# Weight pieces, their loads and three sums moved in a fused attention and feed-forward kernel

## The chip, the cores and the metric

The kernel runs on one core of a Trainium2 chip. The metric is the device time of one execution in microseconds. A core has TensorE (matmuls), VectorE (DVE), ScalarE (ACT), GpSimd (Pool) and SyncE (SP, which here only issues transfers), all running their own queue in order, and 16 DMA engines that they share.

## The reference

Three stages follow one another on 8 batches of 576 tokens and 512 channels. Cut to what matters:

```python
def sm_attn(qq, kk, vv):
    s = scale * np.matmul(qq, kk.transpose(0, 1, 3, 2))
    s = s - np.max(s, axis=-1, keepdims=True)
    a = np.exp(s)
    a = a / (np.sum(a, axis=-1, keepdims=True) + 1e-09)
    return np.matmul(a, vv)
p_packed = sm_attn(p, k, v)              # 32 packed rows per head
x = sm_attn(q, p_packed, p_packed)       # (8, 576, 512) after heads are joined
...
xk = mu_k * x + (1.0 - mu_k) * x_prev    # x_prev: x moved by one token
xr = mu_r * x + (1.0 - mu_r) * x_prev
k = np.maximum(xk @ w_k, 0.0)            # 512 -> 1024
x = 1.0 / (1.0 + np.exp(-(xr @ w_r))) * (k * k @ w_v)
...
h = xt @ U @ V                           # over tokens, rank 32
u = x + h.transpose(0, 2, 1)
out = u + np.maximum(u @ w_ch1, 0.0) @ w_ch2   # 512 -> 2048 -> 512
```

## The kernel before

Every matrix product is done in three passes on a high and a low part of each operand (`_hi`, `_lo`): ScalarE writes the high part, VectorE (for the first weights, Pool) subtracts it to get the low part.

**First part, four groups of three chunks (`chunk_plan`).** A chunk is 384 tokens and has 17 places, its slots: eight k groups (L778), three r groups (L757) and six halves of three v groups (L792), each of twelve matmuls. The batches' attention is laid between them at numbered places. Around them go the mix and split of the next chunk, and for each of the three token tiles of a chunk its split (`x2s`, L868 on ScalarE and L872 on VectorE) and its sum over tokens with U (`g`, L861 on TensorE); `g_evac` takes the sum out. The last group of three chunks (kind LAST) has no attention. It has the transposes of u (`u`), their parts (`us`) and, from `PIECE_ITEMS`, the first 20 weight pieces.

**Weight pieces.** The second layer's weights are needed as seven combinations for a Strassen-like product (`NPROD` = 7, 32 pieces of 128 x 1024 numbers). A piece is loaded into `piece_raw` or `late_raw` (L1210 to L1216, by Pool), Pool makes four sums (L1222 to L1227, `pool_piece`), ScalarE writes the high parts (`ws_hi`, L1248), VectorE the low parts (`ws_lo`, L1253), and SyncE stores 896 KB (`ws_store`, L1345) into `w_parts`. The 20 early pieces have three slots and lie in LAST; `b_loads` waits until they are all stored and then loads V, the sums g and the x tiles. The 12 late ones have two slots and lie in the first half pass of the second part.

**Second part (`pair_plan`).** Five pairs of column blocks, each in two halves g with two layers: 28 products of the first (`m1`, L1036, in order e = 7i + pos) and 28 of the second (`m2`, L1118, e from 28). A product is six matmuls. SyncE loads 256 KB of `w_parts` for each of them into an eleven-deep ring (L1365), which waits for the product 11 before. For the second layer ScalarE (L1136) and VectorE (L1142) split the hidden values three products ahead.

**What sets the order.** It is written out: `first_items`, `chunk_plan`, `pair_plan` give one list of items, and each engine takes from it, in this order, what is its own. So an item's place in the list is its place in the queue of every engine that it uses. Pool alone has its own loop. A late piece is converted at the spots of `LATE_SPOTS`; at each spot come first the store of the piece two before, then the split of the one before, then the conversion:

```python
    for kind, after in (("ws_store", 2), ("ws_lo", 1), ("ws_hi", 0)):
```

**Start.** SyncE issues p, then k's first two parts, then q of batch 0; ScalarE issues k's other two and v. `WEIGHTS_AFTER` puts conversions of the first part's ten weight chunks (`w`) behind attention steps; chunks 0 to 3 are w_k, 4 and 5 w_r, 6 to 9 w_v. Line numbers below are those of the profile of this kernel.

## Time and profile before

| | us |
|---|---|
| median of three runs | 1506.16 (1502.21 to 1509.39) |
| profiled execution | 1503.87 |
| its span | 1501.2 |
| TensorE matmul busy | 1342.2 (89%) |
| VectorE busy | 946.9 (63%) |
| ScalarE busy | 699.6 (47%) |
| Pool busy | 228.6 (15%) |

The granted TensorE clock was 0.959 of full speed on the mean. The span runs from the first to the last instruction; 2.7 us lie around it. Busy shares are a mean over stages with different limits, so the stretches of the rows below are read one by one: attention and the first layer to 693.7 us (the last group of chunks from 531.4), the second part from there on.

### The profile page before, as it was taken

How to read it: one execution, taken by the hardware profiler on the slowest of the kernel's cores; microseconds unless marked ns; L12 is line 12 of the kernel's file. 1: busy time of each engine (PE TensorE's matmuls, PEld its weight loads, DVE VectorE, ACT ScalarE, POOL GpSimd, SP SyncE). 2: the span in 40 equal slices, each digit the busy share in tenths (PEclk: the TensorE clock that was granted, in tenths of full speed). 3: DMA queues.
4: the chain of work that ended last, by engine and by line, in shares of the span. 5: the costliest groups of instructions: out<-in, count | busy, mean ns of one | idle time of the engine just before them, and what ended most of it. 6: DMA issues, size and time to landing. Idle time of an engine off the chain costs nothing.

```text
span 1501.2 us, 21219 instructions
## 1 busy us (share of the span) xinstructions
PE 1342.2 (89%) x7592; PEld 1139.1 (76%) x7592; DVE 946.9 (63%) x1549; ACT 699.6 (47%) x1240; POOL 228.6 (15%) x294
## 2 busy tenths in 40 slices
PE   2379999999999997799666999999999999899997
PEld 1268787788878886587444878888788879799996
DVE  2666668666676756636444486756866586467756
ACT  1445465454445553544322454445544554355543
POOL 2700000000000049813432020001100010011000
PEclk9589999999999999899877999999999999999999
DMA  7733243333322048764855757876687668977986
GB/s 149 175 79 73 67 87 80 80 56 75 73 66 59 8 136 272 233 212 139 273 172 184 241 166 212 235 210 205 174 245 217 204 186 245 256 243 237 265 275 163
DMA packets 372454, 252.47 MB, mean 168 GB/s; under 512 B 249280, under 2 KB 286176, under 8 KB 372352
## 3 DMA queue, kind: packets, MB, share of 16 engines
q1 hardware_dynamic: 361056, 235.58, 55.9%
q0 software_dynamic: 4960, 13.79, 3.0%
q10 hardware_dynamic: 6336, 1.77, 0.5%
q8 instruction: 61, 1.00, 0.3%
q14 instruction: 41, 0.34, 0.1%
HBM read 201.25 MB, written 49.81 MB: 167 GB/s over the span
## 4 chain that ended last, share of the span: by engine, by line
PE 68%; DVE 11%; DMA 6%; SPq 4%; POOL 4%; issue 3%; ACT 3%; ACTq 0%; DVEq 0%; POOLq 0%
PE bank L1036 22%; PE bank L1118 19%; PE bank L778 11%; PE bank L792 7%; PE bank L757 3%; SPq L1288 3%; DVE mixed L730 2%; DMA w_parts<-late_out 2%; DVE hid_parts L1142 2%; DMA w_ring<-w_parts 2%; PE bank L861 1%; PE bank L931 1%; ACT mixed L717 1%; DMA late_raw<-in_moe_w_ch 1%; DVE acc L1161 1%
## 5 line engine op out<-in xcount | busy, mean ns | idle before, releaser
L1118 PE MATMUL bank<-hid_parts,w_ring 128*128 128x512 f32 (+1 forms) x1680 | 373.9, 381 | 41.8 <-DVE hid_parts L1142 30.1
L1118 PEld LDWEIGHTS bank<-hid_parts,w_ring 128*128 128x128 f32 x1680 | 312.2, 194 | 101.9 <-issue 53.8
L1036 PE MATMUL bank<-u_parts,w_ring 128*128 128x512 f32 (+1 forms) x1680 | 357.6, 370 | 13.8 <-ACT hid_raw L1046 6.8
L1036 PEld LDWEIGHTS bank<-u_parts,w_ring 128*128 128x128 f32 x1680 | 307.2, 189 | 54.4 <-issue 15.3
L1142 DVE TENSOR_TENSOR hid_parts<-hid_raw,hid_parts 128x512 fp32r<-128x512 f32 (+1 forms) x280 | 186.5, 673 | 97.0 <-ACT hid_parts L1136 93.6
L1136 ACT ACTIVATE hid_parts<-hid_raw 128x512 fp32r<-128x512 f32 (+1 forms) x280 | 163.2, 587 | 145.4 <-PE bank L1118 142.5
L778 PE MATMUL bank<-xk_hi,wk_hi 128*128 128x384 f32 x384 | 133.4, 347 | 13.5 <-DVE xk_lo L749 8.9
L778 PE MATMUL bank<-xk_lo,wk_hi 128*128 128x384 f32 x384 | 130.9, 341 | 0.0
L778 PE MATMUL bank<-xk_hi,wk_lo 128*128 128x384 f32 x384 | 130.8, 341 | 0.0
L792 PE MATMUL bank<-wv_hi,k_hi 128*128 128x512 f32 x288 | 116.2, 404 | 0.4 <-DVE k_lo L828 0.4
L792 PE MATMUL bank<-wv_lo,k_hi 128*128 128x512 f32 x288 | 114.9, 399 | 0.0
L792 PE MATMUL bank<-wv_hi,k_lo 128*128 128x512 f32 x288 | 114.3, 397 | 0.0
L835 DVE TENSOR_TENSOR square<-square 128x384 f32<-128x384 f32 x96 | 55.3, 576 | 88.6 <-ACT square L812 88.2
L812 ACT ACTIVATE square<-bank 128x384 f32<-128x384 f32 x96 | 46.9, 488 | 114.3 <-PE bank L778 100.9
L1070 DVE TENSOR_TENSOR hid_raw<-bank,hid_raw 128x512 f32<-128x512 f32 (+1 forms) x40 | 25.5, 638 | 112.0 <-PE bank L1036 112.0
L778 PEld LDWEIGHTS bank<-xk_hi,wk_hi 128*128 128x128 f32 x384 | 73.8, 192 | 23.0 <-issue 13.9
L1161 DVE TENSOR_TENSOR acc<-bank,acc 128x512 f32<-128x512 f32 (+1 forms) x140 | 86.4, 629 | 7.2 <-PE bank L1118 6.9
L730 DVE SCALAR_TENSOR_TENSOR mixed<-x,mu,mixed 128x384 f32<-128x384 f32 x96 | 58.2, 668 | 42.5 <-ACT mixed L717 42.4
L960 POOL TENSOR_TENSOR u_sums<-acc 128x512 f32<-128x512 f32 (+1 forms) x10 | 11.7, 1179 | 449.2 <-ACT acc L949 449.2
L1059 ACT ACTIVATE hid_raw<-hid_raw 128x512 f32<-128x512 f32 (+1 forms) x80 | 46.9, 587 | 61.7 <-DVE hid_raw L1070 44.4
L778 PEld LDWEIGHTS bank<-xk_lo,wk_hi 128*128 128x128 f32 x384 | 73.9, 192 | 1.0
L778 PEld LDWEIGHTS bank<-xk_hi,wk_lo 128*128 128x128 f32 x384 | 73.8, 192 | 0.0
(155 smaller groups left out, 1921.7 us busy)
## 6 DMA issues: line engine op xcount, KB each, us to landing
w_ring<-w_parts SPq DMA_DIRECT2D x560, 256.0 KB, 3.7
w_parts<-piece_out SPq DMA_DIRECT2D x20, 896.0 KB, 5.0
w_parts<-late_out SPq DMA_DIRECT2D x12, 896.0 KB, 5.5
x_scratch<-x SPq DMA_DIRECT2D x36, 256.0 KB, 2.0
kq_parts<-in_k SPq DMA_DIRECT2D x120, 72.0 KB, 2.6
kq_parts<-in_q SPq DMA_DIRECT2D x112, 72.0 KB, 2.2
v_rows<-in_v SPq DMA_DIRECT2D x56, 128.0 KB
out_dram<-acc SPq DMA_DIRECT2D x84, 64.0 KB, 3.0
```

The costliest lines, as they stand in the source:

```text
L730: last = nc.vector.scalar_tensor_tensor(out3, segments(c, ft, 0), mu[:, which, ft:ft + 1], out3, ALU.mult, ALU.add)
L757: last = nc.tensor.matmul(bank, a, b_, start=(done == 0), stop=(done == 3 * n_terms - 1))
L778: last = nc.tensor.matmul(bank[:, 0:CHUNK], wk[a][:, ct, at * P:(at + 1) * P], xk[b_][:, ct, :], start=(ct == 0 and a == 0 and b_ == 0), s ...
L792: last = nc.tensor.matmul(bank, k2[a][:, f, at * P:(at + 1) * P], wv[b_][:, f, :], start=(f == 0 and a == 0 and b_ == 0), stop=(f == NFA - ...
L812: nc.scalar.activation(square[:, at % 2, :], bank[:, 0:CHUNK], ACT.Relu).then_inc(k_ev, 1)
L835: nc.vector.tensor_tensor(square[:, at % 2, :], square[:, at % 2, :], square[:, at % 2, :], ALU.mult).then_inc(squared, 1)
L1036: last = nc.tensor.matmul(to, wring[:, e % RW, ct, a, :], uc[:, pos, b, ct, 0:w], start=(pos in FRESH and ct == 0 and a == 0 and b == 0), ...
L1059: nc.scalar.activation(h, h, ACT.Relu).then_inc(relu_ok, 1)
L1118: last = nc.tensor.matmul(role(st, j, BANK_OF[pos])[:, 0:w], wring[:, e % RW, j, a, :], hid[:, no % RH, b, 0:w], start=(pos in FRESH and i ...
L1136: nc.scalar.activation(hid[:, no % RH, 0, 0:w], raw[:, pos, i, 0:w], ACT.Copy).then_inc(hid_hi, 1)
L1142: nc.vector.tensor_tensor(hid[:, no % RH, 1, 0:w], raw[:, pos, i, 0:w], hid[:, no % RH, 0, 0:w].bitcast(F32), ALU.subtract).then_inc(hid_l ...
L1161: nc.vector.tensor_tensor(to, role(st, j, name)[:, 0:w], to, ALU.add).then_inc(sum_ok, 1)
```

## The change

- The 12 late pieces are placed four products apart from e = 3 on: conversion at e, split and store at e + 1. Before, they stood at 14 spots three to five products apart, conversion, split and store one spot after the other.
- The 20 early pieces stand at 3 + 9n/5 instead of 4 + 7n/5, their stores two places after the conversion instead of three, and SyncE issues their loads (`ws_load`) instead of Pool, two pieces ahead. The late pieces are still loaded by Pool, one ahead.
- The sum g of tile 3c+1 moves from the end of its chunk to behind the second k group of the next; the split of tile 3c-1 and its sum go one to three places later. In the last chunk `b_loads`, `b_v`, `u` and `us` start one place later.
- At the start Pool issues the first p load (with a semaphore of its own), ScalarE issues v after the second and the fourth part of k have landed, weight chunks 4 and 5 are converted after the first mix, and Pool's low part of chunk 4 waits for the split of the first mix.

```diff
@@ -74,7 +74,7 @@
...
-WEIGHTS_AFTER = {"scores2": 1, "sm1": 3, "norm1": 2}
+WEIGHTS_AFTER = {"scores2": 1, "sm1": 3}
@@ -126,9 +126,13 @@
...
         items.append(slot)
-        if at == (2 if c == 2 else 0) and (c > 0 or kind != FIRST):
+        if at == (4 if c == 2 else 2) and (c > 0 or kind != FIRST):
             items.append(("x2s", 3 * c - 1, 0) if c > 0 else ("x2s", 8, -1))
-        if c == 2 and at == 1:
+        if at == 1 and (c > 0 or kind != FIRST):
+            items.append(("g", 3 * c - 2, int(c == 0), 0) if c > 0 else ("g", 7, 1, -1))
+            if c == 2:
+                items.append(("g_evac", 0, 0))
+        if c == 2 and at == 3:
             items.append(("g", 4, 1, 0))
@@ -136,16 +140,12 @@
...
                 items += loads_after(n, step)
-        if at == 4 and c == 0 and kind != FIRST:
+        if at == 5 and c == 0 and kind != FIRST:
             items += [("g", 8, 1, -1), ("g_evac", 1, -1)]
-        if at == 3 + c and c > 0:
+        if at == (5 if c == 1 else 7) and c > 0:
             items.append(("g", 3 * c - 1, c - 1, 0))
...
             items.append(("g", 3 * c, int(c == 2), 0))
-        if at == NSLOT - 1:
-            items.append(("g", 3 * c + 1, int(c == 2), 0))
-            if c == 1:
-                items.append(("g_evac", 0, 0))
         if not last_chunk:
@@ -160,11 +160,10 @@
...
-            items += {4: [("b_loads",)], 6: [("b_v",)], 7: [("u", 0, 0), ("u", 0, 1)], 8: [("u", 0, 2), ("u", 0, 3)],
-                      9: [("u", 0, 4), ("u", 0, 5), ("b_ring",)], 10: [("u", 0, 6), ("u", 0, 7)],
-                      11: [("us", 0, 0), ("us", 0, 1)], 12: [("us", 0, 2), ("us", 0, 3)], 13: [("us", 0, 4), ("us", 0, 5)],
-                      14: [("us", 0, 6), ("us", 0, 7)], 15: [("us", 0, 8), ("us", 0, 9), ("us", 0, 10)],
-                      16: [("us", 0, 11), ("us", 0, 12), ("us", 0, 13)]}.get(at, [])
+            us = lambda *ks: [("us", 0, k) for k in ks]
+            items += {5: [("b_loads",)], 7: [("b_v",)], 8: [("u", 0, 0), ("u", 0, 1)], 9: [("u", 0, 2), ("u", 0, 3)],
+                      10: [("u", 0, 4), ("u", 0, 5), ("b_ring",)], 11: [("u", 0, 6), ("u", 0, 7)],
+                      12: us(0, 1), 13: us(2, 3), 14: us(4, 5, 6), 15: us(7, 8, 9), 16: us(10, 11, 12, 13)}.get(at, [])
     return items
@@ -195,10 +194,14 @@
...
     for n in range(PIECES - LATE):
-        at = 4 + 7 * n // 5
+        at = 3 + 9 * n // 5
+        if n == 0:
+            plan.setdefault(0, []).extend([("ws_load", m) for m in range(SLOTS_P)])
+        elif n + SLOTS_P - 1 < PIECES - LATE:
+            plan.setdefault(at, []).append(("ws_load", n + SLOTS_P - 1))
         plan.setdefault(at, []).append(("ws_hi", n))
         plan.setdefault(at + 1, []).append(("ws_lo", n))
-        plan.setdefault(at + 3, []).append(("ws_store", n))
+        plan.setdefault(at + 2, []).append(("ws_store", n))
     return plan
@@ -230,22 +233,18 @@
...
-LATE_SPOTS = [(0, 1, 1), (0, 1, 5), (0, 2, 2), (0, 2, 6), (0, 3, 1), (0, 3, 5)] + [(1, 0, e) for e in range(3, 19, 3)] + [(1, 0, 21), (1, 0, 24)]
+def late_items(e):
+
+
+    n, rest = divmod(e - 3, 4)
+    if e < 3 or n >= LATE or rest > 1:
+        return []
+    n += PIECES - LATE
+    return [("ws_hi", n)] if rest == 0 else [("ws_lo", n), ("ws_store", n)]
...
 TURN_AT = (5, 11, 17, 23)
-
-
-def late_pieces(spot):
-
-
-    at = LATE_SPOTS.index(spot)
-    items = []
-    for kind, after in (("ws_store", 2), ("ws_lo", 1), ("ws_hi", 0)):
-        if 0 <= at - after < LATE:
-            items.append((kind, PIECES - LATE + at - after))
-    return items
@@ -256,8 +255,9 @@
...
                 items.append(("m1", g, i, pos))
-                if p == 0 and g == 0 and i == 0 and pos < 3:
-                    items += [[("x2s", 8, PAIRS - 1)], [("g", 8, 1, PAIRS - 1)], [("g_evac", 1, PAIRS - 1)]][pos]
+                if p == 0 and g == 0 and i == 0 and pos < 4:
+                    items += [[("g", 7, 1, PAIRS - 1)], [("x2s", 8, PAIRS - 1)], [("g", 8, 1, PAIRS - 1)],
+                              [("g_evac", 1, PAIRS - 1)]][pos]
                 if i > 0 and pos < 2:
@@ -267,8 +267,8 @@
...
                     items += turns.pop(0)
-                if p == 0 and g == 0 and (0, i, pos) in LATE_SPOTS:
-                    items += late_pieces((0, i, pos))
+                if p == 0 and g == 0:
+                    items += late_items(NPROD * i + pos)
                 if g == 0 and i == 1 and pos == 0 and p < NB - 1:
@@ -282,8 +282,8 @@
...
             items.append(("m2", g, pos, i))
-            if p == 0 and g == 0 and (1, 0, e) in LATE_SPOTS:
-                items += late_pieces((1, 0, e))
+            if p == 0 and g == 0:
+                items += late_items(NPROD * NU + e)
             if g == 0 and e in TURN_AT and turns:
@@ -356,7 +356,7 @@
...
         self.z_early_in = [sem(f"z_early_in{i}") for i in range(KQ - ZS)]
-        self.p_in, self.v_in = sem("p_in"), sem("v_in")
+        self.p_first_in, self.p_in, self.v_in = sem("p_first_in"), sem("p_in"), sem("v_in")
         self.kq_ok, self.p_scaled, self.pT_ok = sem("kq_ok"), sem("p_scaled"), sem("pT_ok")
@@ -1199,7 +1199,7 @@
...
-    def load_piece(pool, n):
+    def load_piece(eng, n):
@@ -1207,13 +1207,13 @@
...
             rows = w1.rearrange("(k c p) f -> p c k f", k=2, c=2, p=P)[:, half, :, :]
-            pool.dma_start(r[:, 1:5:3, :], rows[:, :, fa:fa + P]).then_inc(piece_in[slot], 16)
-            pool.dma_start(r[:, 0:8:7, :], rows[:, :, fb:fb + P]).then_inc(piece_in[slot], 16)
+            eng.dma_start(r[:, 1:5:3, :], rows[:, :, fa:fa + P]).then_inc(piece_in[slot], 16)
+            eng.dma_start(r[:, 0:8:7, :], rows[:, :, fb:fb + P]).then_inc(piece_in[slot], 16)
         else:
             cols = lambda f: w2[f:f + P, :].rearrange("p (k j n) -> p j k n", k=2, j=2)[:, half, :, :]
-            pool.dma_start(r[:, 1, :], cols(fa)[:, 0, :]).then_inc(piece_in[slot], 16)
-            pool.dma_start(r[:, 0, :], cols(fa)[:, 1, :]).then_inc(piece_in[slot], 16)
-            pool.dma_start(r[:, 4:8:3, :], cols(fb)).then_inc(piece_in[slot], 16)
+            eng.dma_start(r[:, 1, :], cols(fa)[:, 0, :]).then_inc(piece_in[slot], 16)
+            eng.dma_start(r[:, 0, :], cols(fa)[:, 1, :]).then_inc(piece_in[slot], 16)
+            eng.dma_start(r[:, 4:8:3, :], cols(fb)).then_inc(piece_in[slot], 16)
@@ -1226,15 +1226,15 @@
...
-    def pool_pieces(pool, first, end, slots):
-        for n in range(first, first + slots - 1):
-            load_piece(pool, n)
-        for n in range(first, end):
+    def late_pieces(pool):
+        first = PIECES - LATE
+        load_piece(pool, first)
+        for n in range(first, PIECES):
             pool_piece(pool, n)
-            if n + slots - 1 < end:
+            if n + 1 < PIECES:
                 if n > first:
                     pool.wait_ge(piece_lo, n)
-                load_piece(pool, n + slots - 1)
+                load_piece(pool, n + 1)
@@ -1292,7 +1292,7 @@
...
             src = p[n, hp:H:2, :, 32 * dh:32 * dh + 32].rearrange("c n d -> n c d")
-            eng.dma_start(att.pz[32 * quad:32 * quad + 32, :, :], src).then_inc(att.p_in, 16)
+            eng.dma_start(att.pz[32 * quad:32 * quad + 32, :, :], src).then_inc(att.p_in if n else att.p_first_in, 16)
@@ -1328,7 +1328,6 @@
...
-                load_p(sp, 0)
                 for i in range(CT // 2):
@@ -1414,6 +1413,13 @@
...
                     load_ring(e)
+            elif item[0] == "ws_load":
+                if item[1] < SLOTS_P:
+                    sp.wait_ge(att.x_act, 2 * B)
+                    sp.wait_ge(att.x_dve, 2 * B)
+                else:
+                    sp.wait_ge(piece_lo, item[1] - SLOTS_P + 1)
+                load_piece(sp, item[1])
             elif item[0] == "ws_store":
@@ -1461,9 +1467,13 @@
...
-            pool.wait_ge(att.p_in, 64 * (n + 1))
+            if n:
+                pool.wait_ge(att.p_in, 64 * n)
+            else:
+                pool.wait_ge(att.p_first_in, 64)
             nc.gpsimd.tensor_scalar(att.pz[:, :, :], att.pz[:, :, :], SCALE, None, ALU.mult).then_inc(att.p_scaled, 1)
...
+        load_p(pool, 0)
         for i, m in enumerate((mu_k, mu_r)):
@@ -1485,6 +1495,8 @@
...
             pool.wait_ge(w_hi, i + 1)
+            if i == CT:
+                pool.wait_ge(x_lo, 2)
             nc.gpsimd.tensor_tensor(dst[1], parts(stage_a[i % RA], a), dst[0].bitcast(F32),
@@ -1497,13 +1509,14 @@
...
         pool.wait_ge(att.x_dve, 2 * B)
-        pool_pieces(pool, 0, PIECES - LATE, SLOTS_P)
+        for n in range(PIECES - LATE):
+            pool_piece(pool, n)
         pieces_stored(pool)
...
         pool.wait_ge(u_lo, 2 * NPROD)
-        pool_pieces(pool, PIECES - LATE, PIECES, 2)
+        late_pieces(pool)
         for p in range(1, NB):
@@ -1553,6 +1566,8 @@
...
                     load_z(act, 0, i)
+                act.wait_ge(att.z_in[CT // 2 - 1], 64)
+                act.wait_ge(att.z_in[CT - 1], 64)
                 load_v(act, 0)
```

The order on ScalarE in the second layer of the first half pass; late_out is the conversion of a late piece, hid_parts a split. Before:

```order
L1248 ACTIVATE late_out<-late_raw 128x7x128
L1136 ACTIVATE hid_parts<-hid_raw 128x512 x3
L1248 ACTIVATE late_out<-late_raw 128x7x128
L1136 ACTIVATE hid_parts<-hid_raw 128x512 x3
L1248 ACTIVATE late_out<-late_raw 128x7x128
L1136 ACTIVATE hid_parts<-hid_raw 128x512 x3
L1248 ACTIVATE late_out<-late_raw 128x7x128
L1136 ACTIVATE hid_parts<-hid_raw 128x512 x7
```

And now:

```order
L1248 ACTIVATE late_out<-late_raw 128x7x128
L1136 ACTIVATE hid_parts<-hid_raw 128x512 x4
L1248 ACTIVATE late_out<-late_raw 128x7x128
L1136 ACTIVATE hid_parts<-hid_raw 128x512 x4
L1248 ACTIVATE late_out<-late_raw 128x7x128
L1136 ACTIVATE hid_parts<-hid_raw 128x512 x6
```

Four splits instead of three stand between two conversions, and six instead of seven behind the last.

The order on SyncE in the middle of the early pieces, where pieces of w2 are stored: piece_raw is a load, w_parts<-piece_out a store, x_scratch the store of a token tile. Before, where the loads were Pool's:

```order
L1345 DMA w_parts<-piece_out 896x1x256 [waits piece_lo] x2
L1397 DMA x_scratch<-x 128x512 [waits x2_ok]
L1345 DMA w_parts<-piece_out 896x1x256 [waits piece_lo]
L1345 DMA w_parts<-piece_out 128x7x256 [waits piece_lo] x8
L1397 DMA x_scratch<-x 128x512 [waits x2_ok]
```

And now:

```order
L1396 DMA x_scratch<-x 128x512 [waits x2_ok]
L1344 DMA w_parts<-piece_out 896x1x256 [waits piece_lo]
L1214 DMA piece_raw<-in_moe_w_ch 128x128 [waits piece_lo]
L1215 DMA piece_raw<-in_moe_w_ch 128x128
L1216 DMA piece_raw<-in_moe_w_ch 128x2x128
L1344 DMA w_parts<-piece_out 128x7x256 [waits piece_lo]
L1214 DMA piece_raw<-in_moe_w_ch 128x128 [waits piece_lo]
L1215 DMA piece_raw<-in_moe_w_ch 128x128
L1216 DMA piece_raw<-in_moe_w_ch 128x2x128
```

A load stands behind the store of an earlier piece in one queue.

The order on ScalarE at the start, from the second exp of batch 0 on; wk_hi, wr_hi and wv_hi are the weight conversions, x the copy of the attention's result. Before:

```order
L1563 ACTIVATE wk_hi<-stage_x 128x1024
L1563 ACTIVATE wr_hi<-stage_x 128x1024
L1563 ACTIVATE wr_hi<-stage_r 128x1024
L607 ACTIVATE x<-bank 128x2x288 x2
L717 ACTIVATE mixed<-x,one_minus_mu 128x384 x4
L742 ACTIVATE xk_hi<-mixed 128x768 x2
L1563 ACTIVATE wv_hi<-stage_r 128x1024 x2
```

And now:

```order
L1578 ACTIVATE wk_hi<-stage_x 128x1024
L607 ACTIVATE x<-bank 128x2x288 x2
L717 ACTIVATE mixed<-x,one_minus_mu 128x384 x4
L742 ACTIVATE xk_hi<-mixed 128x768 x2
L1578 ACTIVATE wr_hi<-stage_x 128x1024
L1578 ACTIVATE wr_hi<-stage_r 128x1024
L1578 ACTIVATE wv_hi<-stage_r 128x1024 x2
```

The two conversions of w_r moved behind the copies, the mix and its split.

## Rows read from the trace of the kernel before

**Rows 1.** Stretches: length, busy us by engine, PEclk, DMA share, GB/s.

```profile
577.00:642.20 65.20, 51.68 (x230) 43.40 (x230) 43.33 (x51) 30.33 (x50) 53.06 (x76) 0.92 0.78 252
531.40:693.70 162.30, 140.78 (x675) 121.32 (x674) 92.99 (x125) 77.61 (x136) 89.55 (x130) 0.95 0.60 196
693.70:829.40 135.70, 95.44 (x338) 74.17 (x339) 62.88 (x85) 43.23 (x70) 49.32 (x80) 0.84 0.69 216
```

**Rows 2.** Chain that ended last: start us, length, engine, output and line.

```profile
81.75 2.09 DVE mixed L730 x4
...
386.36 10.43 PE bank L778 x60
...
959.03 33.09 PE bank L1118 x144
```

**Rows 3.** Waits, of 693-830, 545-642, 531-694, 185-545: total, times, longest.

```profile
ACT late_out L1248 <- DMA w_parts<-late_out: 63.5, 9, 8.7
...
ACT piece_out L1248 <- POOL piece_raw L1227: 42.1, 15, 4.9
...
PE bank L861 <- DVE x2s_lo L872: 13.8, 3, 6.4
...
PE bank L861 <- DVE x2s_lo L872: 6.6, 3, 3.2
```

**Rows 4.** Timeline of Pool, late pieces: start, length, what, [idle before <- releaser].

```profile
695.64 0.72 POOL L1210 DMA_DIRECT2D late_raw<-in_moe_w_ch  x1 [6.26 <-DVE u_parts L999]
...
702.00 0.72 POOL L1210 DMA_DIRECT2D late_raw<-in_moe_w_ch  x1
...
735.33 0.45 POOL L1222 TENSOR_TENSOR late_raw<-late_raw 128x128 f32<-128x128 f32 x1 [2.98 <-DMA late_raw<-in_moe_w_ch]
...
790.43 0.56 POOL L1214 DMA_DIRECT2D late_raw<-in_moe_w_ch  x1
...
797.39 0.60 POOL L1222 TENSOR_TENSOR late_raw<-late_raw 128x128 f32<-128x128 f32 x1 [5.17 <-DMA late_raw<-in_moe_w_ch]
...
800.52 0.55 POOL L1214 DMA_DIRECT2D late_raw<-in_moe_w_ch  x1
```

**Rows 5.** Early pieces: Pool's timeline, then landing times of stores and loads.

```profile
596.55 0.55 POOL L1214 DMA_DIRECT2D piece_raw<-in_moe_w_ch  x1
...
601.43 0.55 POOL L1214 DMA_DIRECT2D piece_raw<-in_moe_w_ch  x1
...
DMA to landing us min/median/max: 4.2/5.3/8.6
...
DMA to landing us min/median/max: 2.6/4.0/5.3
```

**Rows 6.** Last chunk: timeline of SyncE and TensorE, then landing of x_tiles.

```profile
643.97 0.52 SPq L1345 DMA_DIRECT2D w_parts<-piece_out  x1
...
651.59 0.52 SPq L1382 DMA_DIRECT2D x_tiles<-x_scratch  x1
...
660.14 0.66 PE L931 MATMUL bank<-ident,x_tiles 128*128 128x128 f32 x4 [0.34 <-DVE v L1658]
...
DMA to landing us min/median/max: 5.3/6.5/7.7
```

**Rows 7.** Timeline of the start, all engines.

```profile
6.25 10.15 ACTq L1302 DMA_DIRECT2D v_rows<-in_v  x8
...
17.73 0.71 DVE L632 STREAM_TRANSPOSE kqT<-kq_parts 128x512 f32<-128x512 f32 x1 [6.53 <-DMA kq_parts<-in_k]
...
23.52 0.74 ACT L588 ACTIVATE probs<-bank,neg_max 128x576 f32<-128x576 f32 x1 [2.98 <-DVE neg_max L650]
...
49.67 17.79 SPq L1288 DMA_DIRECT2D kq_parts<-in_k  x16
...
54.70 5.67 DVE L730 SCALAR_TENSOR_TENSOR mixed<-x,mu,mixed 128x384 f32<-128x384 f32 x4 [1.38 <-ACT mixed L717]
...
70.55 1.77 PE L533 MATMUL bank<-kqT,pT 64*32 64x288 f32 x32 [3.43 <-DVE pT L646]
```

## The prediction

> **What bounds the kernel now.** I read the busy time by stretch first. The last group of three chunks (531.4 to 693.7 us) and the first half of the first pass of the second layer (693.7 to 829.4 us) are where TensorE is not full: 140.8 of 162.3 us and 95.4 of 135.7 us, at a granted clock of 0.95 and 0.84 [rows 1]. The chain of waits gives the undisturbed pace: five k groups in 10.43 us, and 144 matmuls of 512 columns in 33.09 us, 0.230 us each [rows 2]. So a chunk of eight k groups and nine groups of twelve 512-column matmuls needs 8 x 2.09 + 9 x 2.76 = 41.5 us and some 1.4 us for three sums, 43 us; three chunks and some 6 us for the transposes of u make 135 us, and the stretch loses 27 us, of which the middle chunk alone (577 to 642, 65.2 us) loses 22. The half pass needs 56 products x 6 x 0.230 = 77 us and loses 58 us.
>
> The waits say why. ScalarE runs in order, and its conversion of a weight piece (L1248) waits: 63.5 us in 9 waits, up to 8.7 us each, for the store of the piece two before it, and 42.1 us in 15 waits for Pool's sums of the piece [rows 3]. Behind it stand ScalarE's evacuations and splits, without which TensorE has no operand or no bank. The x2s waits of TensorE in these chunks (13.8 us, 3 times) come from the same stall; between 185 and 545 us they are 6.6 us.
>
> **Late pieces (12, in the half pass).** Before, piece n's store is issued two places after its conversion, and the conversion of n+2, which needs the same slot, stands right behind it. So every piece pays a landing, 7 us of ScalarE's time on the mean. After, the store stands one product after the conversion and the slot is wanted eight products later; this wait goes. What is late next is Pool: it loads one piece ahead, and issue, landing and four sums follow one another on it. From 695.64 to 702.00 us that took 6.4 us for the first piece; for a w2 piece it took 10.1 us (790.43 to 800.52), made of 1.8 of issue, 5.17 of waiting for the landing and 3.1 of sums [rows 4]. In the lightest case of the same rows the landing leaves 2.98 us of waiting, and a sum takes 0.45 us. Lower bound of the period: 1.8 + 3.0 + 1.8 = 6.6 us; upper bound 10.1. After the change the store of a piece starts some 2 us behind the next load instead of ahead of it, and VectorE is idle when ScalarE waits, so I take 1.8 + 4.2 + 2.4 = 8.4 us. Four products at full speed take 5.5 us, so Pool, not TensorE, sets the pace.
> End of the half pass: first sums done at 702.0; three more w1 pieces at 6.7, 722; eight w2 pieces x 8.4, 789; a conversion, its latency and nine products, 14, gives 803 instead of 829.4: **-26 us** (bounds: period 10.1 gives 817, -12; 6.6 gives 789, -41). A check by bytes: the stage moves 135.7 us x 216 GB/s = 29.3 MB [rows 1]; in 109 us this is 268 GB/s, more than the 252 GB/s which the busiest chunk held for 65 us, so there is little room below 8 us.
>
> **Early pieces (20, in the last three chunks).** Their loads leave Pool for SyncE. Pool's cycle was 4.88 us (596.55 to 601.43) [rows 5], with 1.8 of issue in it; it becomes some 3.1 us, while the pieces come every 1.8 places instead of 1.4: 3.7 us among k groups, 4.9 among r and v. The Pool wait should nearly go, and the x2s waits behind it. I leave 7 us of stall of the 27. Now SyncE has each load behind the store of an earlier piece and behind the waits of the x stores. Nobody else is queued there but the stores themselves; a load has two pieces, over 7 us, of lead.
> The Trainium skill (DMA: Bandwidth & Descriptors, Issuing engines are not separate DMA queues) says that DMAs from all engines share 16 DMA engines, and that another issuing engine saves only issue time. By that rule the move is worth the 1.8 us on Pool and nothing in transfer; a landing is not made shorter by it. The trace cannot show it before the change.
> The price comes at the end. The last piece is stored at place 39 instead of 33, and the loads for the second layer wait until all pieces are stored. Before: store at 643.97, x_tiles issued at 651.59, 7.6 us later, landing 6.5 us, and TensorE's first use at 660.14, some 2 us after that [rows 6]. After: four more k groups and the conversion put the last store 14 us behind the chunk's start (642.2 in the trace); +7.6 + 6.5 gives 28 us behind it, while its use stands 20.7 us behind it (660.14 - 642.2 and one r group more). TensorE waits 7 to 8 us, and restarts slowly; I take 9. With 1 us for the tighter splits of u: 27 - 7 - 9 - 1 = **-10 us**. The other way round: the first piece is split 8 us after 531.4, the last one 20 periods later, then come 14 us to x_tiles and 31 us to the first product (660.14 to 693.7, one r group less). With today's 4.88 us that is 8 + 98 + 45 = 151 us, 11 less than now. Bounds: -20 (2 us of stall in the chunks, 6 at the end, no more) and +3 (5.6 us a piece, 165 us).
>
> **Middle sums.** The sums of tile 3c+1 move from the end of a chunk behind the second k group of the next, and the splits two places later. Nothing is added; ScalarE's and VectorE's work is the same. Of the 6.6 us of [rows 3] and a little before 185 us I take **-5**, bounds 0 and -7: VectorE's attention steps can be as late at the new place.
>
> **Start.** The v loads of batch 0 now wait on ScalarE until two z loads have landed, and its first exp is queued behind them. Eight of the ten took 10.15 us to issue, so some 13 us in all [rows 7]. The last k of batch 0 was there at 17.73 with v's packets beside it; without them I take 13. Then ScalarE is free near 26 instead of 19, and exp starts at some 27 instead of 23.52: +3.5. The first p load moves to Pool, whose next work waits anyway. Against it: one weight conversion that waited for its DMA stood before the copy of x (-1.6), and the mix took 5.67 us for four operations while Pool worked beside it, against 2.09 at 81.75 [rows 2] (-3.5). What Pool now does later still ends before its reader.
> The Trainium skill (SBUF — State Buffer, Who interferes with whom) says that a VectorE operation with two SBUF inputs and a GpSimd operation that reads SBUF lock each other out. The row agrees, and by the rule the whole 3.5 us are won at that place.
> But TensorE then meets batch 1's scores, which wait for its k; they start at 70.55, three us behind the end of k's issue on SyncE (49.67 + 17.79) [rows 7]. That issue stands behind batch 0's q and batch 1's v, and v waits for batch 0's pv, which comes 2 to 4 us later. So the gain is not seen at all, and the loss partly, as the transfers still have the same bytes to move: **+1 us**, bounds -4 and +5.
>
> **Sum.** -26 - 10 - 5 + 1 = -40. The profiled execution took 1503.87 us (span 1501.2, 2.7 around it); it becomes 1464. The median before, 1506.16, is 2.3 above it, so I predict 1465 to 1466: **1465 us**.
>
> **The rivals.** A, Pool's late cycle stays at 10.1 us because loads and stores still meet: -12 instead of -26, **1479**. For it: the last five w2 pieces all had it. Against: in those the store was issued first.
> B, the late pieces run at 6.6 us: -41 instead of -26, **1450**. For it: the light landings. Against: the bytes, 29.3 MB in 95 us, 308 GB/s.
> C, slower than before. SyncE's queue serialises the early pieces: store landing 5.3, then the load behind it 4.0 [rows 5], sums 3.1 to 4, conversion and split 2.3, is 15.2 us a round. With three pieces a round that is 5.1 us, near today's. If only two are in flight (load n+2 is issued beside conversion n) it is 7.6 us a piece: 8 + 152 + 45 = 205 us for the stretch instead of 162. That is +43 - 26 - 5 + 1 = +13, **1519**. It decides from some 7 us a piece. Against it: three slots, and the load needs only the split of piece n-1.
> D, no change to be told: all bounds on the bad side at once, -12 + 3 + 0 + 5 = -4, **1502**.
> By the Trainium skill (DMA: Bandwidth & Descriptors, Queues, rings and completion order) a ring is consumed in order, and different rows take turns; that speaks for C's mechanism, since the load now shares the store's row.
>
> **How the numbers follow.** Forecast 0.52 (its own range 1453 to 1478: late period 7.6 to 9.3 us is -32 to -19, early stretch 5 either way); A 0.20; B 0.16; C 0.06; D 0.06. The range 1443 to 1490 leaves out C, D and a rest of B. A measurement of this kernel tells 0.5% (7.5 us) from no change. Faster by more: forecast, A and B, 0.88. Within: D, 0.06. Slower: C, 0.06.
>
> **What would show it.** Right: ScalarE's wait for late_out on the stores gone, in its place a wait for Pool's late sums of some 3 us a piece; late conversions 8 to 9 us apart; the second half of the pass starting some 26 us sooner behind the first product; the middle chunk of the last group near 47 us; TensorE waiting once, 5 to 10 us, for x_tiles; the first scores of batch 1 within 3 us of 70.55. Wrong: conversions at 6 or at 10 us (B, A); ScalarE still waiting for Pool in the early pieces, with Pool waiting for a load behind a store (C); a start more than 5 us away.

## The result and the profile after

| | before | after |
|---|---|---|
| median of the executions | 1506.20 us | 1462.90 us |
| lowest and highest | 1502.21 to 1509.39 | 1459.35 to 1465.13 |
| span of the profiled execution | 1501.2 us | 1463.1 us |

The ratio after to before is 0.9712, with a 95% interval from 0.9681 to 0.9742: 2.9% faster, 43.3 us by the medians. The forecast was 1465 us. The two profiled executions stand 38.1 us apart: that of before lies under its median, that of after over its own (it took 1465.13 us).

The sum came out well, but two of its four terms did not. I go through the stretches first. The columns are length, busy us of PE, PEld, VectorE, ScalarE and GpSimd, granted clock, DMA share and GB/s. In the kernel after, the last three chunks one by one (each from its first k product to that of the next, the third up to the first product of the second layer), then the half pass up to the first product of the second half:

```profile
537.87:580.50 42.63, 42.63 (x211) 37.82 (x210) 31.34 (x41) 24.53 (x42) 23.77 (x32) 1.00 0.64 198
580.50:624.89 44.39, 42.89 (x211) 37.74 (x210) 35.30 (x46) 26.21 (x44) 26.29 (x39) 1.00 0.86 272
624.89:688.79 63.90, 52.04 (x258) 45.23 (x256) 26.31 (x40) 26.57 (x49) 18.58 (x21) 0.91 0.56 184
688.79:792.90 104.11, 87.15 (x340) 66.04 (x341) 61.02 (x86) 44.01 (x70) 44.87 (x80) 0.94 0.90 290
```

The kernel before, cut at the same instructions:

```profile
530.87:582.81 51.94, 44.54 (x211) 38.67 (x210) 31.06 (x44) 25.34 (x44) 31.16 (x52) 0.93 0.56 183
582.81:642.01 59.20, 47.34 (x211) 40.20 (x210) 38.35 (x47) 27.87 (x46) 47.35 (x70) 0.91 0.76 245
642.01:693.70 51.69, 49.43 (x258) 42.98 (x256) 24.01 (x37) 24.39 (x47) 11.55 (x10) 1.00 0.47 150
```

With [rows 1] for the half pass of before, the account is: the first two chunks 24.1 us shorter (51.94 + 59.20 against 42.63 + 44.39), the third 12.2 us longer, the half pass 31.6 us shorter; and all of it starts 7.0 us later than before (537.87 against 530.87). Part of the gain shows as a higher granted clock: TensorE's busy time fell by 6.4 us in the first two chunks (0.93 and 0.91 before, 1.00 now) and by 8.3 us in the half pass (0.84 before, 0.94 now), for about the same number of matmuls. These rows also correct the cut of the prediction: it let the middle chunk begin at 577, but its first k product is at 582.8. The loss of 27 us over the three chunks stands; it lay 9 us in the first and 16 us in the middle one, not 22 in the middle.

What ScalarE waits for in the half pass (689 to 793) and in the last three chunks (537 to 689), and TensorE between 185 and 530 us; columns: total, times, longest. They answer to [rows 3].

```profile
ACT late_out L1248 <- POOL late_raw L1227: 29.8, 11, 5.4
...
ACT piece_out L1248 <- POOL piece_raw L1227: 22.6, 11, 3.3
...
PE bank L861 <- DVE x2s_lo L872: 6.6, 3, 3.2
```

The 63.5 us in which a late conversion waited for a store are gone; in their place stand 29.8 us for GpSimd's late sums. GpSimd's timeline shows that round, as [rows 4] did before (start, length, what; in the fences below also, in brackets, the idle time ahead of it and its releaser):

```profile
697.30 0.72 POOL L1210 DMA_DIRECT2D late_raw<-in_moe_w_ch  x1
...
721.49 0.57 POOL L1214 DMA_DIRECT2D late_raw<-in_moe_w_ch  x1
...
774.33 0.56 POOL L1214 DMA_DIRECT2D late_raw<-in_moe_w_ch  x1
```

From 721.49 to 774.33 lie seven w2 pieces: 52.84 / 7 = 7.55 us each. From 697.30 to 721.49 lie three w1 pieces: 8.06 us each.

The last chunk answers to [rows 6]; SyncE and TensorE there:

```profile
640.51 0.51 SPq L1344 DMA_DIRECT2D w_parts<-piece_out  x1
...
646.75 1.16 SPq L1385 DMA_DIRECT2D g<-g_scratch  x2
648.02 0.52 SPq L1381 DMA_DIRECT2D x_tiles<-x_scratch  x1
...
654.52 1.09 PE L931 MATMUL bank<-ident,x_tiles 128*128 128x128 f32 x4 [8.65 <-DMA g<-g_scratch]
```

And the start, all engines, as [rows 7]:

```profile
10.34 9.84 ACTq L1302 DMA_DIRECT2D v_rows<-in_v  x8
...
13.07 2.18 PE L533 MATMUL bank<-kqT,pT 64*32 64x288 f32 x32 [13.07 <-DVE pT L646]
...
24.38 0.74 ACT L588 ACTIVATE probs<-bank,neg_max 128x576 f32<-128x576 f32 x1
...
30.49 2.36 PE L550 MATMUL bank<-v_rows,probs 128*32 128x64 f32 x80 [2.83 <-DMA v_rows<-in_v]
...
55.03 4.43 DVE L730 SCALAR_TENSOR_TENSOR mixed<-x,mu,mixed 128x384 f32<-128x384 f32 x4 [1.38 <-ACT mixed L717]
...
72.36 4.67 POOL L1500 TENSOR_TENSOR wv_lo<-stage_x,wv_hi 128x1024 fp32r<-128x1024 f32 x2
...
72.98 4.94 DVE L835 TENSOR_TENSOR square<-square 128x384 f32<-128x384 f32 x2
73.11 2.17 PE L533 MATMUL bank<-kqT,pT 64*32 64x288 f32 x32 [5.43 <-DVE pT L646]
...
79.30 0.74 ACT L588 ACTIVATE probs<-bank,neg_max 128x576 f32<-128x576 f32 x1 [1.29 <-DVE neg_max L650]
```

The z loads of batch 0 (here the parts of k) now land first, and the first scores start at 13.07 us instead of 20.46. But the first exp starts at 24.38, later than before, pv (the product with v) at 30.49 instead of 26.73, and batch 1's scores at 73.11. The last sum of x in the first chunk starts at 137.34 us instead of 131.42. GpSimd's last weight part, VectorE's squares and batch 1's exp in the kernel before, for comparison with the last rows:

```profile
66.97 4.64 POOL L1488 TENSOR_TENSOR wv_lo<-stage_x,wv_hi 128x1024 fp32r<-128x1024 f32 x2
...
70.42 2.08 DVE L835 TENSOR_TENSOR square<-square 128x384 f32<-128x384 f32 x2
...
73.88 0.74 ACT L588 ACTIVATE probs<-bank,neg_max 128x576 f32<-128x576 f32 x1 [1.29 <-DVE neg_max L650]
```

### The profile page after: what moved, and what is told of

The parts are those of the page before. It is cut to its first block, busy times and chain, and to the rows that moved or that the text cites. A ratio compares the mean times of both kernels' runs of the same rounds, so it can differ in the third digit from the quotient of the medians.

```text
span 1463.1 us, 21223 instructions
## 1 busy us (share of the span) xinstructions
PE 1332.2 (91%) x7592; PEld 1130.9 (77%) x7592; DVE 944.6 (65%) x1549; ACT 700.4 (48%) x1240; POOL 200.3 (14%) x250
## 4 chain that ended last, share of the span: by engine, by line
PE 64%; DVE 13%; DMA 9%; SPq 4%; POOL 3%; issue 3%; ACT 2%; ACTq 1%; DVEq 0%; POOLq 0%
PE bank L1036 21%; PE bank L1118 18%; PE bank L778 9%; PE bank L792 7%; PE bank L757 4%; DMA late_raw<-in_moe_w_ch 4%; DVE mixed L730 2%; DMA w_ring<-w_parts 2%; SPq L1288 1%; DVE hid_parts L1142 1%; PE bank L931 1%; DVE square L835 1%; DVE u_parts L999 1%; SPq L1302 1%; DMA piece_raw<-in_moe_w_ch 1%
## 5 line engine op out<-in xcount | busy, mean ns | idle before, releaser
L1118 PE MATMUL bank<-hid_parts,w_ring 128*128 128x512 f32 (+1 forms) x1680 | 361.4, 371 | 20.2 <-DVE hid_parts L1142 11.4
L1118 PEld LDWEIGHTS bank<-hid_parts,w_ring 128*128 128x128 f32 x1680 | 301.6, 188 | 78.5 <-issue 33.9
L835 DVE TENSOR_TENSOR square<-square 128x384 f32<-128x384 f32 x96 | 59.0, 616 | 80.3 <-ACT square L812 80.1
```

The lines of the kernel that those rows point to most:

```text
L835: nc.vector.tensor_tensor(square[:, at % 2, :], square[:, at % 2, :], square[:, at % 2, :], ALU.mult).then_inc(squared, 1)
L1118: last = nc.tensor.matmul(role(st, j, BANK_OF[pos])[:, 0:w], wring[:, e % RW, j, a, :], hid[:, no % RH, b, 0:w], start=(pos in FRESH and i ...
```

## The experiments

My theory after the two traces: each of the four parts of the change works in its own stretch, and they add up, -32, -12, 0 and +5 or 6 us. The rival: the parts are entangled (a faster clock, other transfers, a sum moved by another edit). So first each part was undone alone. The times of before in these runs had medians of 1504.7 to 1506.6 us, so that medians can be compared across runs.

### Late pieces undone

```diff
-                if p == 0 and g == 0:
-                    items += late_items(NPROD * i + pos)
+                if p == 0 and g == 0 and (0, i, pos) in LATE_SPOTS:
+                    items += late_pieces((0, i, pos))
```

> The changed kernel with the twelve late pieces back at their old places (store two places behind the conversion, the next conversion of the slot right behind it); all else as changed. Read from the two traces, the late half pass lost 31.5 of its 136.6 us, so the local theory gives 1462.9 + 31.5 = 1494, with ScalarE's waits for the stores back at some 60 us. The prediction's own term (26) gives 1489. The rival is that part of the 31.5 us is the gift of something else (the faster clock of a fuller stretch before, or loads of the second layer that now come in another order): then under 20 us come back, 1482 or less.

Measured: 1495.81 us, ratio to before 0.9933 (0.991 to 0.9957). That is 32.9 us more than the changed kernel. Its half pass, and ScalarE's wait in it:

```profile
684.05:821.18 137.13, 96.84 (x340) 75.07 (x341) 63.04 (x86) 43.36 (x70) 49.68 (x80) 0.84 0.68 215
```

```profile
ACT late_out L1252 <- DMA w_parts<-late_out: 62.7, 9, 8.7
```

The stretch is back at its old length, clock and wait, with the chunks ahead of it still in their new form. The late term is 33 us and comes from this edit alone.

### Early pieces undone

```diff
-        at = 3 + 9 * n // 5
+        at = 4 + 7 * n // 5
...
-        for n in range(PIECES - LATE):
-            pool_piece(pool, n)
+        pool_pieces(pool, 0, PIECES - LATE, SLOTS_P)
```

with the stores, the loads on GpSimd and the places of u as before.

> The changed kernel with the twenty early pieces back as before: their loads on GpSimd, 1.4 places apart, store three places behind, and u of the last chunk one place sooner. Read from the traces, the last three chunks went from 162.3 to 149.9 us: 12.4 us should come back, 1475. The prediction's term (10) gives 1473. The rival: the last three chunks gained because the sums of the middle tile moved, not by the pieces; then less than 5 us come back here and the 12 us appear in the run with the sums undone.

Measured: 1478.25 us, ratio 0.9819 (0.9789 to 0.9849), 15.4 us more than the changed kernel. In its own trace the last three chunks take 164.7 us (539.43 to 704.10) against 150.9, that is 13.8 us; the cut above, against the kernel before, gave 11.9 (24.1 less 12.2). The differences are within the intervals. ScalarE's wait for GpSimd's sums is 42.7 us in 15 waits again.

### Early loads back on GpSimd, places as changed

```diff
-        elif n + SLOTS_P - 1 < PIECES - LATE:
-            plan.setdefault(at, []).append(("ws_load", n + SLOTS_P - 1))
...
+        pool_pieces(pool, 0, PIECES - LATE, SLOTS_P)
```

> The changed kernel with one part of the early pieces' edit undone: their loads are issued by GpSimd again, two pieces ahead; the places of conversions, splits and stores stay as changed (1.8 places apart). Undoing the whole edit cost 15.3 us (1478.3 against 1462.9). Theory 1, what was won is GpSimd's time (1.8 us of issue in a round of 4.9): most of it goes again, 1472 to 1478, and ScalarE waits for the sums as long as before (some 40 us). Theory 2, it is the wider spacing, and the queue that issues is of no account: 1463 to 1466. In between tells the shares.

Measured: 1470.38 us, ratio 0.9761 (0.974 to 0.9782): 7.5 us of the 15.4 go again. ScalarE's wait in the last three chunks, here and below it in the kernel with the whole part undone:

```profile
ACT piece_out L1244 <- POOL piece_raw L1223: 32.7, 15, 3.9
```

```profile
ACT piece_out L1245 <- POOL piece_raw L1224: 42.7, 15, 5.0
```

42.7 us with both undone, 32.7 with the new places, 22.6 with the new places and SyncE: each half of the edit takes 10 us off the wait and some 7.5 off the time. In the traces the three chunks take 164.7, 159.0 and 150.9 us. Neither theory alone was right; the shares are about equal. (The half called places holds the earlier stores and the later u too.) That the move to another queue bought GpSimd's issue time, 1.8 us a piece, fits this but is argued, and it is not the whole of it, for GpSimd now waits more for landings: 2.6 us in 4 waits with the loads in its own queue, and in the changed kernel (the window takes in the wait for the first piece of all)

```profile
POOL piece_raw L1222 <- DMA piece_raw<-in_moe_w_ch: 165.6, 14, 130.0
```

so that 35.6 us in 13 waits remain beside the first, of 130.0.

### Middle sums undone

```diff
-        if at == (4 if c == 2 else 2) and (c > 0 or kind != FIRST):
+        if at == (2 if c == 2 else 0) and (c > 0 or kind != FIRST):
...
+        if at == NSLOT - 1:
+            items.append(("g", 3 * c + 1, int(c == 2), 0))
```

> The changed kernel with the middle tile's sums and the splits of x2 at their old places. By the prediction's term (5 us won) it would take 1468. By the trace, where the milestones between 185 and 530 us drifted by +1.5 us and the waits for x2s there stayed at 6.6 us in 3 waits, the move is worth nothing in that stretch: 1461 to 1463, unless the last three chunks need it.

Measured: 1462.12 us, ratio 0.971 (0.9682 to 0.9737), 0.8 us less than the changed kernel: nothing. The last sum of x in two successive chunks, first the changed kernel, then this one:

```profile
245.98 0.69 DVE L846 TENSOR_TENSOR x<-bank,x 128x512 f32<-128x512 f32 x1 [0.77 <-PE bank L792]
...
297.56 0.69 DVE L846 TENSOR_TENSOR x<-bank,x 128x512 f32<-128x512 f32 x1 [0.54 <-PE bank L792]
```

```profile
245.36 0.69 DVE L845 TENSOR_TENSOR x<-bank,x 128x512 f32<-128x512 f32 x1 [2.16 <-PE bank L791]
...
296.05 0.69 DVE L845 TENSOR_TENSOR x<-bank,x 128x512 f32<-128x512 f32 x1 [0.54 <-PE bank L791]
```

And its wait for x2s from 185 to 530 us:

```profile
PE bank L860 <- DVE x2s_lo L871: 6.6, 3, 3.2
```

The chunk takes 51.58 us with the move and 50.69 without (before: 50.68); the same 0.9 us shows again at the next middle group. From the last sum of x in the first chunk to that in the ninth, 400.7 us pass with the move and 400.9 without it, so even this is made up elsewhere. The waits of TensorE for x2s from 185 to 530 us are 6.6 us in 3 waits in all three kernels: the move did not touch the waits it was credited with.

### Start undone, and its wait alone

```diff
-WEIGHTS_AFTER = {"scores2": 1, "sm1": 3}
+WEIGHTS_AFTER = {"scores2": 1, "sm1": 3, "norm1": 2}
...
-            if i == CT:
-                pool.wait_ge(x_lo, 2)
...
-                act.wait_ge(att.z_in[CT // 2 - 1], 64)
-                act.wait_ge(att.z_in[CT - 1], 64)
```

with the first p load on SyncE again. In the second kernel only the last two lines are taken out.

> The changed kernel with the start as before: weight parts in their old order, no wait of ScalarE for z ahead of the v loads, no wait of GpSimd for x_lo, first p load on SyncE. By the prediction's term (+1) it takes 1462. By the traces the third tile of the first chunk was summed at 137.3 instead of 131.4 us and the lag stayed: undoing it gives 6 us, 1457. The rival: the lag is made up later by slack elsewhere, and nothing is won.

> The changed kernel without ScalarE's two waits for z ahead of the v loads of batch 0; the other edits of the start stay. Undoing all of the start took 5.2 us off (1457.7 against 1462.9). Theory 1, the wait is the cost: nearly all comes back, 1458, the first exp starts when the scores are there (within 3 us of their end), pv near 27 us. Theory 2, the cost is in the order of the weight parts and GpSimd's wait for x_lo, which is still running when batch 1's k is wanted: 1462 to 1463.

Measured: 1457.72 us, ratio 0.9681 (0.9652 to 0.9711), with the whole start undone; 1458.71 us, ratio 0.9693 (0.9672 to 0.9715), with the wait alone taken out. The start costs 5.2 us and 4.2 of them are the wait, by medians whose intervals reach 3 to 5 us to either side. The rows show where the time goes. The second kernel:

```profile
68.32 4.64 POOL L1500 TENSOR_TENSOR wv_lo<-stage_x,wv_hi 128x1024 fp32r<-128x1024 f32 x2
...
71.86 1.99 DVE L835 TENSOR_TENSOR square<-square 128x384 f32<-128x384 f32 x2
71.99 2.18 PE L533 MATMUL bank<-kqT,pT 64*32 64x288 f32 x32 [9.00 <-DVE pT L646]
...
75.23 0.74 ACT L588 ACTIVATE probs<-bank,neg_max 128x576 f32<-128x576 f32 x1 [1.29 <-DVE neg_max L650]
```

Batch 1's scores come only 1.1 us sooner than in the changed kernel, but the exp behind them 4.1 us sooner (75.23 against 79.30). Between them stands VectorE's pair of squares: 1.99 us here, 4.94 in the changed kernel, where GpSimd's wv_lo runs from 72.36 to 77.03 beside it. In this kernel wv_lo ends at 72.96. The pair ends 0.9 us behind the end of wv_lo in both (77.92 and 73.85). So of the 4.1 us at that exp, 1 is the direct cost of the wait, by the later v, k and scores, and 3 come because GpSimd's weight parts are moved into the way of VectorE. That these 4.1 us are the 4.2 of the time is not shown: single traces scatter by more between there and the end of the chunk (see what is still open).

### v of batch 0 on GpSimd, in two places

```diff
-                act.wait_ge(att.z_in[CT // 2 - 1], 64)
-                act.wait_ge(att.z_in[CT - 1], 64)
-                load_v(act, 0)
...
+        pool.wait_ge(att.z_in[CT // 2 - 1], 64)
+        pool.wait_ge(att.z_in[CT - 1], 64)
+        load_v(pool, 0)
```

> The changed kernel with the v loads of batch 0 issued by GpSimd, behind the first p load and the same two waits for z, instead of by ScalarE. ScalarE is then free when the scores of batch 0 are there. If the loss of the start is ScalarE's queue behind the wait, and not the order of the packets, the first exp starts near 17 to 18 us instead of 24.4, pv follows v's landing near 22 to 25 instead of 30.5, and the loss of 5.2 us goes with a gain of some 2 more: 1455 to 1458. If it is the packets of v, which land as late as before, pv stays near 30 and the time at 1462.

> As the run with v's loads on GpSimd, but placed behind the scaling of the first p, which there stood behind them and held back the first scores to 22.2 us. If ScalarE's queue is what the wait costs, the scores start near 13, the first exp near 16 to 17, pv as soon as v has landed, 24 to 27 instead of 30.5, and the time is 1454 to 1458. If the start is bound by the bytes (batch 1's k and the weights are behind v in any case), the scores and exp come sooner and the time stays at 1461 to 1463.

Measured: 1461.57 us, ratio 0.9707 (0.9688 to 0.9727), where v's loads stand ahead of GpSimd's small loads and its scaling of p; the scores started at 22.23 us only, since the scaling of p was queued behind v. My expectation of an exp at 17 us fell by that, and the run did not test what it was meant to. With the loads behind the scaling: 1457.98 us, ratio 0.9677 (0.9654 to 0.9699). Its start:

```profile
16.03 0.74 ACT L592 ACTIVATE probs<-bank,neg_max 128x576 f32<-128x576 f32 x1 [8.53 <-DVE neg_max L654]
...
66.51 4.66 POOL L1507 TENSOR_TENSOR wv_lo<-stage_x,wv_hi 128x1024 fp32r<-128x1024 f32 x2
...
67.81 4.24 DVE L839 TENSOR_TENSOR square<-square 128x384 f32<-128x384 f32 x2
...
73.44 0.74 ACT L592 ACTIVATE probs<-bank,neg_max 128x576 f32<-128x576 f32 x1 [1.29 <-DVE neg_max L654]
```

With nothing else queued behind the wait, the order z before v brings everything forward at first: scores at 12.96, exp at 16.03, pv at 24.95, and the issue of batch 1's k starts at 45.81 instead of 51.60. But the squares are still caught behind wv_lo (4.24 us), and the time equals that of the old start: no gain over it is shown.

### Late loads on SyncE, two pieces ahead

```diff
-    return [("ws_hi", n)] if rest == 0 else [("ws_lo", n), ("ws_store", n)]
+    return [("ws_hi", n)] if rest == 0 else [("ws_lo", n), ("ws_load", n + 2), ("ws_store", n)]
...
-            if n + 1 < PIECES:
-                if n > first:
-                    pool.wait_ge(piece_lo, n)
-                load_piece(pool, n + 1)
```

> The changed kernel with the loads of the twelve late pieces issued by SyncE, two pieces ahead (each behind the split of the piece two before it), so that GpSimd only sums. Theory 1, GpSimd's serial round (issue, landing, sums: 7.55 us by the trace) sets the late pace: the period falls to TensorE's four products, 5.5 to 6 us, and the half pass from 105 to some 90 us, 1448 to 1450. Theory 2, the bytes set it (29.3 MB in 105 us is 279 GB/s already): the period stays over 7 us, 1457 to 1463, and GpSimd waits as long for landings as before.

Measured: 1447.97 us, ratio 0.9622 (0.9604 to 0.964), 14.9 us less than the changed kernel. The half pass, ScalarE's waits for a late conversion, and the page's line on the late stores (KB each, median us to landing):

```profile
686.52:778.35 91.83, 83.39 (x341) 66.00 (x342) 62.02 (x86) 45.09 (x70) 29.61 (x48) 0.95 0.98 328
```

```profile
ACT late_out L1244 <- DMA w_parts<-late_out: 5.5, 2, 5.0
ACT late_out L1244 <- POOL late_raw L1229: 4.1, 3, 2.2
```

```profile
w_parts<-late_out SPq DMA_DIRECT2D x12, 896.0 KB, 7.2
```

The stretch is 12.3 us shorter, and ScalarE's wait for GpSimd falls from 29.8 to 4.1 us. GpSimd's first sums of the eight w2 pieces lie between 721.0 and 764.6 us, 6.2 us apart. Theory 1 holds, if with a period of 6.2 us where it said 5.5 to 6: the serial round on GpSimd set the late pace, not the bytes. The rate rose to 328 GB/s over the stretch; a late store now lands after 7.2 us instead of 5.2, a late load after 4.2 instead of 3.8. Here the Trainium skill (DMA: Bandwidth & Descriptors, Issuing engines are not separate DMA queues) fits what was seen: another engine saves issue time and no transfer time. The landings got longer, not shorter, and the gain is the round that GpSimd no longer has to serve one step after the other. The run changes two things at once, the queue that issues and the lead (two pieces instead of one); no run parts them.

### 22 early pieces instead of 20

```diff
-LATE = 12
+LATE = 10
...
-        at = 3 + 9 * n // 5
+        at = 3 + 8 * n // 5
```

> The changed kernel with 22 pieces in the last three chunks and 10 in the half pass, instead of 20 and 12: the early ones stand 1.6 places apart instead of 1.8, and end at the same place. By the trace two late pieces of 7.55 us go, 15 us; an early round of GpSimd is near 3.1 us and two more should cost 0 to 6 us: 1448 to 1454. The rival: the early stretch is at its limit too (in which case ScalarE waits for GpSimd's sums there again, by more than the present 22.6 us), and gives back 10 us or more: 1458 or above.

Measured: 1469.68 us, ratio 0.9774 (0.9746 to 0.9801), 6.8 us more. The time is the rival's (1458 or above), and so is ScalarE's longer wait. The three chunks and the half pass, then two waits in the chunks:

```profile
534.53:694.31 159.78, 138.98 (x677) 121.09 (x676) 91.56 (x127) 79.12 (x137) 65.62 (x98) 0.95 0.68 217
694.31:792.87 98.56, 86.33 (x340) 66.81 (x341) 59.05 (x84) 42.12 (x68) 38.55 (x68) 0.93 0.89 282
```

```profile
ACT piece_out L1248 <- POOL piece_raw L1227: 31.2, 12, 5.7
...
PE bank L861 <- DVE x2s_lo L872: 8.6, 2, 6.9
```

The chunks take 159.8 us instead of 150.9, the half pass 98.6 instead of 104.1. That is 3.3 us of the 6.8; the profiled execution is this kernel's fastest (1465.34 us) and enters the chunks 3.3 us sooner than that of the changed kernel. My expectation of 15 us less there was reckoned wrongly: without a late piece its four products still take 5.5 us, so that a piece costs 7.55 - 5.5 = 2 us, and two of them 4. With pieces 1.6 places apart GpSimd waits 47.7 us in 13 waits for landings (35.6 in 13 in the changed kernel), ScalarE waits longer for the sums, and TensorE again waits up to 6.9 us for x2s. The spacing of 1.8 is near the edge.

### The two best together, and three products apart

> The changed kernel with the late pieces' loads on SyncE, two ahead (15 us won alone), and the start as before (5 us won alone). The two stretches are over 500 us apart, so the two should add up: 1448.0 - 5.2 = 1443. If the lag of the start is partly absorbed later on, 1446 to 1448.

Measured: 1443.30 us, ratio 0.9584 (0.9559 to 0.9608): the two gains add up to within a us. This kernel beats both. In it the late pieces were then set three products apart:

```diff
-    n, rest = divmod(e - 3, 4)
+    n, rest = divmod(e - 3, 3)
```

> The kernel of the run before (late loads on SyncE, start as before, 1443.3 us) with the twelve late pieces three products apart instead of four. There the period ran at 5.5 to 7 us with 350 to 380 GB/s moved, where the changed kernel moved 280 to 335. Theory 1, the transfers are now what binds: the pieces come no faster, TensorE only waits sooner, 1441 to 1446. Theory 2, four products of 5.5 us still set the pace: the pieces end some 10 us sooner and the half pass, which is still 10 us over its unhindered 77, gives back 3 to 8: 1435 to 1440.

Measured: 1456.20 us, ratio 0.967 (0.9647 to 0.9693), 12.9 us slower; both theories missed the size and the second the sign. The half pass has 10.5 us of it. That stretch, the same of the kernel it was made from, and the wait that came back:

```profile
678.03:777.87 99.84, 85.83 (x340) 67.05 (x341) 63.62 (x86) 44.57 (x70) 29.33 (x48) 0.91 0.93 302
```

```profile
681.12:770.42 89.30, 81.47 (x341) 63.98 (x341) 61.37 (x86) 44.81 (x70) 29.65 (x48) 0.98 0.99 337
```

```profile
ACT late_out L1244 <- DMA w_parts<-late_out: 16.7, 6, 5.8
```

Two slots three products apart leave six products for conversion, split and landing of a store, eight before. ScalarE stands in its queue for the store again, 16.7 us, as it did in the kernel before with 63.5.

## Why the prediction was right, and where it was not

**Late pieces: -26 predicted, -31.6 in the trace, -32.9 by undoing.** The mechanism was the one forecast: the wait for the store vanished, and a wait for GpSimd's sums took its place, 29.8 us over 11 pieces, 2.7 each (some 3 forecast). Mis-sized was the period: 8.4 us predicted, 7.55 measured for w2, eight of them 7 us less. Two smaller errors largely cancel each other: the three w1 pieces took 8.06 instead of 6.7 us (+4), the tail from the last sums to the second half 11.3 instead of 14 (-3). What misled me was the check by bytes. I took 252 GB/s, which the busiest chunk held for 65 us, as near the ceiling. It was a mean over a stretch, and shorter stretches of the kernel before already spoke against it:

```profile
693.70:750.00 56.30, 42.66 (x176) 34.07 (x176) 26.03 (x36) 23.04 (x38) 23.29 (x41) 0.91 0.81 264
...
710.00:715.00 5.00, 5.00 (x24) 4.14 (x23) 3.66 (x6) 3.33 (x6) 0.82 (x2) 1.00 1.04 388
```

The changed half pass then ran at 290 GB/s, and at 328 with the loads on SyncE. The floor near 8 us did not exist, and rival B's "308 GB/s" was no argument against it. B (1450) was missed because of GpSimd's round, not because of the bytes.

**Early pieces: -10 predicted, -11.9 in the trace, -15.4 by undoing.** Both sides of the term were in the right place. The stall fell by 24 us (20 forecast), and the price at the end was 12.2 us (10 forecast): the wait of 8.65, 2.6 us more of busy time at a granted clock of 0.91 (52.04 against 49.43, where 1 us was reckoned for the slow restart), and 1 of the rest. The last store stands 15.6 us behind the chunk's start (14), x_tiles is issued 7.5 us after it (7.6), and the first use comes 29.6 us behind the start (28); TensorE waited 8.65 us (7 to 8). The trace puts that wait down to g, not to x_tiles. But the two loads of g were issued by 647.91 and none of the kernel took over 5.8 us to land, while an x_tiles load took 5.8 to 7.6: the last one to land before 654.52 was x_tiles, as forecast. By half the gain comes with the loads on SyncE, by half with the new places; the prediction had not parted them. Rival C, a queue of SyncE that serialises, did not come as a loss, but its sign was there in part: GpSimd does wait for loads now, 35.6 us in 13 waits, and ScalarE's wait for the sums, which should nearly have gone, is still 22.6 us. With a lead of two pieces this no longer holds up TensorE: its first two chunks take 87.0 us, where the prediction reckoned 86 without a stall.

**Middle sums: -5 predicted, nothing measured (+0.8 by undoing, within the noise).** The step that failed is the first: I credited the move with the x2s waits between 185 and 545 us, 6.6 us in 3 waits, without having shown that these waits hang on the middle tile. They are the same in the kernel after. The bound (0) held. Two chunks even take 0.9 us more, and the eight chunks behind the first together the same.

**Start: +1 predicted with bounds -4 and +5; +5.2 by undoing, +5.9 in the pair of traces.** The direct part was read rightly: pv 3.8 us later (2 to 4 forecast), batch 1's scores 2.6 us later (within 3). Exp came at 24.38, sooner than the 27 I had, and that changed nothing. The sentence that failed is "What Pool now does later still ends before its reader". I asked only who reads what GpSimd writes, not who runs beside it. I had counted the collision at the mix as a gain of 3.5 us: it went down from 5.67 to 4.43 only, as GpSimd's wk_lo (55.10, 2.36 us) still runs beside it (and to 2.21 in the kernel without the wait, where nothing does). And I had not looked at the other one: GpSimd's last weight part lay over VectorE's squares before already, but only from 70.42 to 71.61; ending 5.4 us later, it now covers them from 72.98 to 77.03, and neg_max and batch 1's exp are queued behind them. That exp is 5.4 us later (79.30 against 73.88), of which the scores explain 2.6 and the longer squares (4.94 against 2.08) the rest. The rule from the Trainium skill (SBUF — State Buffer, Who interferes with whom) was cited in the prediction for the gain at one place; by the same rule the loss at the other could have been found.

**Sum.** By undoing: -32.9 - 15.4 + 0.8 + 5.2 = -42.3, against 43.3 measured. The forecast of 1465 for 1462.9 owes much to luck: the two pieces' terms were 12.3 us too cautious by undoing (7.5 by the traces), the sums and the start 10 us too kind. The chosen mechanisms were right in the two terms that carry nine tenths of the forecast gain (36 of 40 us), and wrong in the other two.

**Still open.** Up to batch 1's exp the profiled kernels with the changed start agree within 2 us (78.2 to 80.1), but their last sum of x in the first chunk starts at 132.2, 132.4, 134.7, 134.7, 134.9, 137.3 or 137.3 us: steps of 2.5 us that no edit explains. The four kernels with the old start show the same scatter, 126.7, 129.3, 129.3 and 131.4 us. I have not found what decides it. It is why a single trace is not enough for a term of 5 us at the start; the means of the seven and the four, 134.8 and 129.2, are 5.6 us apart and bear the term out. Nor was it tried whether GpSimd's last weight parts can be kept clear of the squares with z still loaded first; my estimate from the squares (4.24 us there, 0.56 each alone) is some 3 us at that place.

## What to carry to other kernels

When a wait for a landing is taken out of an in-order engine's queue, write down the next serial loop, step by step on the engine that serves it; its issue, landing and work add up until one of them goes to another queue, and that round (7.55 us here) was worth another 15 us. A rate that a kernel held over a long stretch is a mean of what it asked for (252 GB/s here, with 388 over 5 us in the same profile): don't make a floor for a period of it. For every operation that is moved in time, look not only for its reader but for what it will now run beside, above all VectorE with two operands in SBUF beside GpSimd, and show that a wait hangs on the moved step before crediting the move with it.
